# Gate columns on a second load queue, an early table load, and the batch-1 sigmoid one slot sooner, in an mLSTM plus mixer kernel

## The reference, cut to what matters

```python
def _attn_ref(q, k, v, i_gate, f_gate, o_gate):      # B, H, S, D = 4, 8, 768, 40
    ...
    for t in range(S):
        m_new = np.maximum(f_gate[:, :, t] + m, i_gate[:, :, t])
        f_stab = np.exp(f_gate[:, :, t] + m - m_new)
        i_stab = np.exp(i_gate[:, :, t] - m_new)
        m = m_new
        C = f_stab[..., None, None] * C + i_stab[..., None, None] * outer(vt, kt)
        n = f_stab[:, :, None] * n + i_stab[:, :, None] * kt
        h_tilde = C @ qt
        denom = np.maximum(np.abs(sum(n * qt)), 1.0)
        o = 1.0 / (1.0 + np.exp(-o_gate[:, :, t]))
        y[:, :, t] = o * h_tilde / denom

def _moe_ref(x, w_tok1, w_tok2, w_ch1, w_ch2):       # x is y as (4, 768, 320)
    h = np.maximum(xt @ w_tok1, 0.0) @ w_tok2        # over tokens, 768 -> 256 -> 768
    u = x + h.transpose(0, 2, 1)
    h2 = np.maximum(u @ w_ch1, 0.0) @ w_ch2          # over channels, 320 -> 1536 -> 320
    return u + h2
```

## Time and profile before

| | |
|---|---|
| device time, median of 3 runs | 464.92 us (463.87 to 465.5) |
| device time of the profiled execution | 465.76 us |
| its span | 464.0 us |
| granted clock of PE, mean over the span | 0.993 of full speed |
| busy: PE / PEld / DVE / ACT / POOL | 443.6 / 410.5 / 257.6 / 209.6 / 206.6 us |
| chain of waits that ended last, by engine | PE 88%, DVE 4%, issue 2%, ACT 2%, DMA 1% |

### The profile page before, as it was taken

How to read it: one execution, slowest core, us unless ns; L and a number is a source line. 1 busy time by engine, 2 the same in 40 slices (tenths; PEclk the granted TensorE clock), 3 DMA queues, 4 the chain that set the end, 5 groups by cost and what they waited for, 6 DMA issues and landing times.

```text
span 464.0 us, 9523 instructions
## 1 busy us (share of the span) xinstructions
PE 443.6 (96%) x3471; PEld 410.5 (88%) x3471; DVE 257.6 (56%) x592; ACT 209.6 (45%) x516; POOL 206.6 (45%) x293
## 2 busy tenths in 40 slices
PE   6999989799999998999999998999999998999996
PEld 2687878789999997899999997989999997999996
DVE  6879964567765437677674227577674325222212
ACT  3565447656555246755552226855552213211120
POOL 6623510578887234698872204598874000000000
PEclk9899999899999999999999999999999999999999
DMA  7547991044444412544444012444410010000101
GB/s 214 189 136 210 332 261 55 17 137 124 140 131 158 133 49 87 148 129 139 130 159 132 10 43 86 139 129 132 140 60 1 1 42 1 0 2 0 45 1 42
DMA packets 36520, 47.38 MB, mean 102 GB/s; under 512 B 3324, under 2 KB 28986, under 8 KB 36474
## 3 DMA queue, kind: packets, MB, share of 16 engines
q1 hardware_dynamic: 35674, 45.79, 32.5%
q10 hardware_dynamic: 800, 0.98, 0.7%
HBM read 42.73 MB, written 4.03 MB: 101 GB/s over the span
## 4 chain that ended last, share of the span: by engine, by line
PE 88%; DVE 4%; issue 2%; ACT 2%; DMA 1%; POOL 0%; DVEq 0%; SPq 0%; POOLq 0%
PE pC L1147 32%; PE pS L1059 7%; PE pA L1218 7%; PE pA L1219 7%; PE pA L1220 7%; PE pY L1116 5%; PE pA L1147 4%; PE pA L1223 3%; PE pA L1222 3%; PE pY L1095 2%; PE pN L1071 2%; DMA u<-i_gate_dram 1%; PE pA L1177 1%; PE pC L1059 1%; PE pC L1106 1%
## 5 line engine op out<-in xcount | busy, mean ns | idle before, releaser
L968 DVE SCALAR_TENSOR_TENSOR h_lo<-pA,h_hi 128x384 fp32r<-128x384 f32 x96 | 53.5, 557 | 154.7 <-ACT h_hi L750 154.7
L750 ACT ACTIVATE h_hi<-pA 128x384 fp32r<-128x384 f32 x96 | 46.9, 489 | 144.5 <-PE pA L1223 144.3
L1147 PE MATMUL pC<-wc_hi,h_hi 128*128 128x320 f32 x288 | 94.4, 328 | 0.8 <-DVE wc_lo L835 0.8
L1147 PE MATMUL pC<-wc_lo,h_hi 128*128 128x320 f32 x288 | 89.0, 309 | 0.0
L1147 PE MATMUL pC<-wc_hi,h_lo 128*128 128x320 f32 x288 | 88.8, 308 | 0.0
L490 POOL TENSOR_TENSOR gb<-gb,pb 128x384 f32<-128x384 f32 (+1 forms) x54 | 52.3, 968 | 59.3 <-ACT pb L620 58.8
L1218 PE MATMUL pA<-uT_hi,wc_hi 128*128 128x384 f32 x192 | 65.6, 342 | 1.9 <-DVE uT_hi L946 1.9
L1219 PE MATMUL pA<-uT_lo,wc_hi 128*128 128x384 f32 x192 | 65.0, 339 | 0.0
L1220 PE MATMUL pA<-uT_hi,wc_lo 128*128 128x384 f32 x192 | 64.6, 337 | 0.0
L1147 PEld LDWEIGHTS pC<-wc_hi,h_hi 128*128 128x128 f32 x288 | 54.2, 188 | 2.1 <-DVE h_lo L968 1.1
L1147 PEld LDWEIGHTS pC<-wc_lo,h_hi 128*128 128x128 f32 x288 | 54.5, 189 | 0.1
(11 more groups left out here) (128 smaller groups left out, 880.6 us busy)
## 6 DMA issues: line engine op xcount, KB each, us to landing
gb<-g_dram SPq DMA_DIRECT2D x18, 512.0 KB, 3.9
kv<-kvN_dram SPq DMA_DIRECT2D x24, 324.0 KB, 3.8
kd<-kT_dram SPq DMA_DIRECT2D x24, 180.0 KB
qz<-qT_dram SPq DMA_DIRECT2D x72, 60.0 KB
out_dram<-u SPq DMA_DIRECT2D x24, 160.0 KB, 1.9
qd<-qT_dram SPq DMA_DIRECT2D x20, 180.0 KB, 2.5
gq<-g_dram SPq DMA_DIRECT2D x45, 60.0 KB
wc_raw<-w_ch_dram SPq DMA_DIRECT2D x6, 384.0 KB, 5.8
```

Source lines behind the costliest of these rows:

```text
L750: nc.scalar.activation(h2[0][:, slot % 2], pA[slot % 2][:, 0:HALF], ACT.Relu).then_inc(h2_hi, 1)
L968: nc.vector.scalar_tensor_tensor(h2[1][:, slot % 2], pA[slot % 2][:, 0:HALF], 0.0, h2[0][:, slot % 2].bitcast(F32), ALU.max, ALU.subtract) ...
L1147: ins = mm(dst, a[p], b[q], start=first and n == 0, stop=last and n == 2)
```

## The change

It has three parts.

1. **Gates.** The first segment (128 columns) of both gates is loaded by ACT, ahead of its output-gate loads; SP loads the other 640 columns. Each half has its own semaphore. DVE waits for the first half alone before `gate_maxima(0)`, fills `carry` after that scan, and then waits for the second half.
2. **Table.** ACT runs a sigmoid on one column of `ident` before it waits for batch 0's output gate, so that the table load stands ahead of the wait.
3. **Slots of batch 0.** `sigmoid(1)` moves from slot 2 to slot 1. `attention(1, -1)` moves from slot 2, behind the sigmoid, to before slot 0. The weight pieces 9 to 15 move one slot later each; 7 and 8 stay in slot 0.

```diff
-SECOND_SIGMOID_AT = 2
+SECOND_SIGMOID_AT = 1
...
-        gates_in = sem("gates_in")
+        gates_in = [sem(f"gates_in{n}") for n in range(2)]
...
-        SLOT_OF_PIECE = [0, 0, 1, 1, 3, 4, 5, 7, 9]
+        SLOT_OF_PIECE = [0, 0, 2, 2, 4, 5, 6, 8, 10]
...
         @block.sync
         def _(sp):
-            sp.dma_start(f_row, f_gate).then_inc(gates_in, 16)
-            sp.dma_start(i_row, i_gate).then_inc(gates_in, 16)
+            sp.dma_start(f_row[:, L:S], f_gate[:, L:S]).then_inc(gates_in[1], 16)
+            sp.dma_start(i_row[:, L:S], i_gate[:, L:S]).then_inc(gates_in[1], 16)
...
+            act.dma_start(f_row[:, 0:L], f_gate[:, 0:L]).then_inc(gates_in[0], 16)
+            act.dma_start(i_row[:, 0:L], i_gate[:, 0:L]).then_inc(gates_in[0], 16)
             o_tiles = o_gate[0, :, :].rearrange("(c p) d -> p c d", p=L)
             for i, (first, last) in enumerate(O_PARTS):
                 act.dma_start(x[:, first:last], o_tiles[:, first:last]).then_inc(o_in[i], 16)
+            act.wait_ge(ident_ready, 2)
+            nc.scalar.activation(den[:, 1:2], ident[:, 0:1], ACT.Sigmoid)
             sigmoid(0)
...
+                if b == 0:
+                    attention(1, -1)
                 for slot in range(SLOTS):
...
                     if more and slot == (SECOND_SIGMOID_AT if b == 0 else 0):
                         sigmoid(b + 1)
-                    if more and step_in(b, slot) >= -1:
+                    if more and step_in(b, slot) >= 0:
                         attention(b + 1, step_in(b, slot))
...
             nc.vector.memset(qz[:, :, :, :, :], 0.0).then_inc(mem_ready, 1)
-            nc.vector.memset(carry, 1.0)
             link(nc.vector.memset(m_row[:, 0:1], 0.0))
-            link(nc.vector.memset(carry.rearrange("p (c t) -> p c t", t=L)[:, :, 0:1], 0.0))
-            dve.wait_ge(gates_in, 32)
...
+            dve.wait_ge(gates_in[0], 32)
             gate_maxima(0)
+            link(nc.vector.memset(carry, 1.0))
+            link(nc.vector.memset(carry.rearrange("p (c t) -> p c t", t=L)[:, :, 0:1], 0.0))
+            dve.wait_ge(gates_in[1], 32)
             gate_maxima(1)
```

## The result

| | before | changed |
|---|---|---|
| device time, median | 464.76 us (461.82 to 466.49, 14 runs) | 461.34 us (460.2 to 463.75, 14 runs) |
| ratio, 95% interval | | 0.9936 (0.9912 to 0.996) |
| profiled execution: time, span | 465.76, 464.0 us | 461.42, 459.7 us |
| its mean granted clock | 0.993 | 0.995 |

The change makes the kernel 0.6% faster, 3.4 us of the 6.3 that I had forecast. The time lies just above the range of 457.3 to 461.0: the direction was right, the size was not. Three runs of the case, at 478, 542 and 864 us, are left out of every ratio and every mean.

The account below looks back on a forecast made before the run. PE's chain was taken to bound the kernel, through two pauses (2.6 and 2.8 us) and the slow clock behind each. Start 1.9 plus slots 4.4 gave 6.3, so 464.92 - 6.3 = 458.6 us, range 457.3 to 461.0.

Parts of the forecast that it names:

- the 6.3: Whole forecast gain in us: 1.9 at the start plus 4.4 in batch 0's slots.
- Gates: DVE at the start: first scan at 3.7, second at 5.2, gate sums at 6.2, 1.8 us sooner than before.
- Rival 2: Start: the second half of the gates lands no sooner, gaining 0.8 instead of 1.9; 459.7 us, chance 0.2.
- ACT at the start: Output gate lands at 7.6, table load no longer follows it, ready for the first exponentials at 11.1.
- I take 1.9: Gain in us at the start, with PE reaching spread_decays(2) at 12.2 or held by ACT's 12.0; ends 0.8 and 2.1.
- What must hide the sigmoid: Slot 1, ACT: batch 1's gate lands at 73.1, sigmoid ends at 76.2, h_hi(2) is 0.2 late, PE doesn't wait.
- Slot 5's slack of 0.3: Piece 12 for hidden(6) is ready at 87.8 and PE comes at 88.1; called the tightest place.
- Piece 14 leaves slot 7, piece 15 comes to slot 10: plus and minus the same: Batch 0's slots: slot 7, where late values cost PE 0.39, is relieved, slot 10 is loaded; no net effect.
- 0.1 for the tight places: Deduction in us from the 4.5 gained in batch 0's slots, for new waits there.
- The term of 4.4: Gain in us in batch 0's slots: 4.5 of stall and clock fall less 0.1; ends 3.2 and 4.9.
- rival 3: Slots 4 to 8: DVE and ACT fall behind PE at full clock, giving back 1.5 to 2; 460.4 us, chance 0.14.
- 1.7 of clock at 86: Loss in us from PE's mean clock of 0.57 from 86 to 90, behind slot 4's wait; booked as gain.

Follow-up runs that it names:

- the slots: Part 3 of the change alone (batch 0's slots), on the kernel before: 461.74 us, ratio 0.9923.
- the stall filled: Kernel before with 13 idle matmuls on PE while it waits for the scores in batch 0's slot 4: 463.71 us, ratio 0.9977.
- the head alone: Parts 1 and 2 of the change (gates and early table load) on the kernel before, run twice: 465.1 us, ratio 0.9985, and 464.56 us, 0.9996.
- the one of the experiments: The kernel before run again unchanged for a second profile: 465.52 us, ratio 1.0008.
- its second profile: The changed kernel run again unchanged for a second profile: 461.7 us, ratio 0.9925 against the kernel before.
- the old slots with fillings: Changed kernel with weight pieces 11 to 15 in slots 3, 4, 5, 7, 9 and idle matmuls at the batch changes: 460.28 us, ratio 0.9902.

## Why the prediction was wrong

**Gates: right.** The first scan at 3.63 (3.7 taken), the second at 5.01 (5.2), the sums at 5.73 (6.2), SP's half landed in time. Rival 2 did not come. The Trainium skill's rule on queues that take turns ("DMA: Bandwidth & Descriptors", section "Queues, rings and completion order") showed no price here: SP's 80 KB loads landed 1.9 and 2.1 us after their issue, with ACT's 960 KB issued right behind them. That doesn't speak against the rule, for at 31 GB/s just behind these landings the large loads had hardly begun.

**ACT at the start: right within 0.3.** Landing 7.90 (7.6), first exponentials 11.34 (11.1). Taking the early table load out moved them by 1.74, 0.45 of it by a later landing.

**PE at the start: the step "I take 1.9" failed.** `spread_decays(2)` came at 12.28, as I said, and the profile pair shows 2.05 at the first `h_hi`. But the base of that difference, 14.03, held a clock fall that the same kernel doesn't have at each execution: 12.84 without it. Of the 1.9, 1.2 was that fall, and of this 1.2 only 0.55 reaches the first `h_hi` (70.85 against 70.30). In profiles without a fall before it, the first `h_hi` stands at 69.96 to 70.41 for the kernels with the old head and at 68.72 to 69.57 for those with the new one, 1.1 us apart in the mean. On top of the slots, the runs without a stretch show only 0.5 (461.28 of 4 runs, 460.74 of 8), good to some 0.3.

**What must hide the sigmoid: right, but closer than I had it.** I put the landing of batch 1's gate at 73.1 on the old trace's scale. It was 71.89, which with the head's 2.05 is 73.9 on that scale, and `h_hi(2)` was 1.0 late in place of 0.2. PE waited for none of it, and the Exp load came behind `h_hi(3)`. The table loads took 1.28 each, with the next activation 0.01 to 0.02 later, so the rows hold against the Trainium skill's 2.66 ("ScalarE: Activation LUTs", section "What ACT_TABLE_LOAD costs"). By slot 5 the pair shows 4.63 us, where I had 4.5. Slot 5's slack of 0.3 became a wait of 0.27, mostly because the piece took 1.33 and not 0.96.

**"Piece 14 leaves slot 7, piece 15 comes to slot 10: plus and minus the same": failed.** I looked for waits at the semaphores and took DVE's durations as fixed. But the 0.39 that slot 7's `values` cost before hung on the clock fall (with the stall filled it is not there), so nothing was won; and in slot 10 the piece's 0.86 and 0.64 more in step 8's chain made PE wait 1.01. With the 0.4 ahead of `hidden(6)` this gives back 1.6 us, where the sum has 0.1 for the tight places. The term of 4.4 was 2.8 + 1.7 - 0.1; measured against the profiled execution it is 3.1 + 2.1 - 1.6, the 3.5 that the pair shows at slot 23. The give-back was rival 3 by its size (460.4), but it has another cause: not PE at full clock, for before with its stall filled runs the same slots at full clock and doesn't pay.

**The clock in the sum: failed.** The 6.3 holds 1.7 of clock at 86 and the 1.2 hidden in 14.03, 2.9 in all, as if each run of before lost them and no run after lost any. The runs show 2.2 lost before and 1.0 after, so 1.2 won. The other 3.4 (2.7 of stall, 0.7 of head) stand against 2.0. So of the 3.1 us missing between the means, 1.7 is clock that I booked and 1.4 is mostly weight pieces; and subtracting it all from a median of three runs carried a single execution's falls into the forecast.

**Open.** What the head adds on top of the slots is not settled. The runs without a stretch say 0.5, while the profiles of the two kernels are 1.5 us apart at slot 23 and 1.3 at the end, once the stretch at 284 is taken off. Some of it goes to waits for DVE and for loads of `qz` in batch 0's attention, which differ between executions. The kernel with the head alone has two stretches or more in 15 of 24 runs and the kernel before in 42 of 83, which is not a clear difference. What sets off the stretches at batch changes was not found. That POOL's company is what stretches DVE's operations is read from rows side by side; no run took POOL's work away, and the 0.96 beside another POOL operation says that not each of them does it.

## What to carry to other kernels

Before a stall's clock fall goes into a sum, look whether a second execution of the same kernel has it; then compare runs with equal mean clock, and book the falls apart. When work is moved out of a stall, check not only that each piece has a wait-free slot but which long operations of the neighbouring engine it will run beside, and try moving fewer things: here sigmoid, step 0 and two pieces were enough for the stall, and in the profiles the five later pieces cost more in their new slots than they brought (49.5 against 48.9). A table load ahead of a wait is cheap and was worth 2.4 us between the means here, half of it by fewer clock falls.

## What was not expected of the hardware

The same 19 matmuls at the start took different times in two executions of before, and 5.58 to 7.21 us over all profiles. First the one that the prediction read, then the one of the experiments:

```profile
1.60 5.61 PE L995 MATMUL pC<-ident 128*128 128x512 bf16 x19 [1.60 <-POOL ident L433]
```

```profile
1.59 6.98 PE L995 MATMUL pC<-ident 128*128 128x512 bf16 x19 [1.59 <-POOL ident L433]
```

The granted clock read 1.00 in both. This sets how long PE stands still before its transposes (2.60 or 1.11), and only behind the longer pause did the clock fall. The length of the pause doesn't decide it, though. At `spread_decays(2)` the changed kernel paused for 1.68 and, in its second profile, for 2.19 us, with no fall behind either, while the old slots with fillings had this at the same place:

```profile
12.52 0.28 PE L1031 MATMUL pA<-above,eye 128*128 128x256 bf16 x1 [1.74 <-ACT gb L672]
```

```profile
12.80:16.00 3.20, 3.20 (x11) 1.16 (x9) 1.71 (x4) 0.95 (x4) 1.27 (x2) 0.50 0.94 289
```

And half-clock stretches came at the changes of batches, at 178 to 184 and 284 us, behind pauses of 0.69 and 0.76 us, in some executions and not in others.
